# Loading each piece of expert weights in two partition halves, each behind a wait on TensorE's progress

## What is computed

```python
def _attn_ref(r, k, v, w, u):          # (4, 8, 768, 48)
    state = zeros((B, H, D, D))
    for t in range(S):
        cur = einsum('bhd,bhe->bhde', u[None] * kt, vt)
        y[:, :, t] = einsum('bhd,bhde->bhe', rt, state + cur)
        state = w[None, :, :, None] * state + einsum('bhd,bhe->bhde', kt, vt)

def _moe_ref(x, phi, w1, w2):          # x (3072, 384), 8 experts, 4 slots each, F = 1024
    logits = x @ phi
    slot_input = softmax(logits, over tokens).T @ x
    slot_out[e] = relu(slot_input[e] @ w1[e]) @ w2[e]
    return softmax(logits, over slots) @ slot_out

def _moe2_ref(x, w_in, w_out):         # d_ff = 2048
    h = x @ w_in
    return max(0.01 * h, h) @ w_out
```

## Time and profile before

| | us |
|---|---|
| median of 3 runs | 419.22 |
| the runs | 416.3 to 419.42 |
| the profiled execution | 414.55 |
| its span, from the first to the last instruction | 412.8 |
| mean granted clock of TensorE, share of full speed | 0.962 |

### The profile page before, as it was taken

The page is one execution under the profiler, slowest core; times in us unless marked ns, Lnnn a source line. Parts: engine busy times, 40 slices in busy tenths (PEclk is TensorE's granted clock), DMA queues, the critical chain, the costliest instruction groups (busy, mean ns, idle before and its releaser), DMA issues.

```text
span 412.8 us, 11083 instructions
## 1 busy us (share of the span) xinstructions
PE 393.9 (95%) x4307; PEld 358.3 (87%) x4307; DVE 252.5 (61%) x435; ACT 230.3 (56%) x601; POOL 58.2 (14%) x73
## 2 busy tenths in 40 slices
PE   8799998989996899989999999999999999999996
PEld 8788998989995344359999999999999999999995
DVE  7987985579863520177856555555555565555553
ACT  5556554256653224767865565565565555655652
POOL 5445453335530100000000000000000000000000
PEclk9789997599999799989999999999999999999999
DMA  7989998689987998900001010010010010100101
GB/s 170 266 247 300 271 272 237 172 244 274 254 302 276 389 402 325 417 32 2 0 2 57 2 57 1 2 57 2 0 58 0 3 54 1 59 0 2 57 2 57
DMA packets 16253, 54.95 MB, mean 133 GB/s; under 512 B 2640, under 2 KB 6224, under 8 KB 15184
## 3 DMA queue, kind: packets, MB, share of 16 engines
q1 hardware_dynamic: 16064, 54.27, 40.6%
q10 hardware_dynamic: 144, 0.05, 0.0%
HBM read 49.60 MB, written 4.72 MB: 132 GB/s over the span
## 4 chain that ended last, share of the span: by engine, by line
PE 91%; issue 3%; DVE 2%; ACT 1%; DMA 1%; SPq 0%; POOL 0%; ACTq 0%; POOLq 0%
PE ps L1009 17%; PE ps L1014 17%; PE ps L1010 16%; PE ps L776 6%; PE ps L987 5%; PE ps L819 5%; PE ps L813 4%; PE ps L797 3%; PE ps L946 3%; PE ps L786 3%; PE ps L927 3%; PE ps L843 2%; PE ps L833 2%; PE ps L890 2%; DMA rk<-rk_t 1%
## 5 line engine op out<-in xcount | busy, mean ns | idle before, releaser
L1009 PE MATMUL ps<-w_hi,g_hi 128*128 128x384 f32 x384 | 131.8, 343 | 0.7 <-ACT g_hi L750 0.7
L1010 PE MATMUL ps<-w_lo,g_hi 128*128 128x384 f32 x384 | 130.0, 339 | 0.0
L603 DVE SCALAR_TENSOR_TENSOR g_full<-h_full 128x384 f32<-128x384 f32 x128 | 71.5, 558 | 89.4 <-ACT h_full L741 89.2
L750 ACT ACTIVATE g_hi<-g_full 128x384 fp32r<-128x384 f32 x128 | 67.3, 526 | 74.4 <-DVE g_full L603 74.0
L1014 PE MATMUL ps<-w_hi,g_lo 128*128 128x384 f32 x384 | 89.2, 341 | 0.0
L1009 PEld LDWEIGHTS ps<-w_hi,g_hi 128*128 128x128 f32 x384 | 72.2, 188 | 1.7 <-ACT g_hi L750 1.0
L1010 PEld LDWEIGHTS ps<-w_lo,g_hi 128*128 128x128 f32 x384 | 72.4, 189 | 0.5 <-issue 0.5
L592 DVE TENSOR_TENSOR g_lo<-g_full,g_hi 128x384 fp32r<-128x384 f32 x128 | 70.5, 551 | 0.1
L741 ACT ACTIVATE h_full<-ps 128x384 f32<-128x384 f32 x128 | 62.4, 487 | 14.4 <-PE ps L987 4.0
L1014 PEld LDWEIGHTS ps<-w_hi,g_lo 128*128 128x128 f32 x384 | 69.6, 189 | 0.0
L661 ACT ACTIVATE bonus_v<-nat,bonus 128x48 f32<-128x48 f32 x192 | 46.0, 322 | 0.8
(11 more groups left out here) (120 smaller groups left out, 354.2 us busy)
## 6 DMA issues: line engine op xcount, KB each, us to landing
w_units<-early_pieces SPq DMA_DIRECT2D x24, 512.0 KB, 6.5
rk<-rk_t SPq DMA_DIRECT2D x48, 192.0 KB, 3.9
nat<-rkv SPq DMA_DIRECT2D x20, 384.0 KB, 5.6
m_unit<-late_units SPq DMA_DIRECT2D x3, 1536.0 KB, 7.1
x_unit<-late_units SPq DMA_DIRECT2D x3, 1536.0 KB, 9.8
out<-y_out SPq DMA_DIRECT2D x7, 576.0 KB, 3.0
w_units<-late_units SPq DMA_DIRECT2D x2, 1536.0 KB, 8.5
m_unit<-w_in SPq DMA_DIRECT2D x4, 768.0 KB, 10.8
```

The lines of the kernel that those rows point to most:

```text
L603: dve.scalar_tensor_tensor(out=g_full[:, f % 2], in0=h_full[:, f % 2], scalar=0.01, in1=h_full[:, f % 2], op0=ALU.mult, op1=ALU.max).then_ ...
L750: act.activation(g_hi[:, f % 4], g_full[:, f % 2], ACT.Copy).then_inc(g_hi_done, 1)
L1009: pe.matmul(bank, g_hi[:, f % 4, bass.ts(s, P)], w_hi[:, f], start=(f == 0), stop=False)
L1010: pe.matmul(bank, g_hi[:, f % 4, bass.ts(s, P)], w_lo[:, f], start=False, stop=False)
```

## The change

A piece is no longer loaded by one DMA on 128 partitions but by two, for partitions 0 to 63 and for 64 to 127, of 256 KB each. In iteration i SP waits ahead of the first half until PE has finished the scores of step i-3, and ahead of the second until it has finished the bonus sums of step i-3. The four pieces after the loop are issued as eight halves without waits. The count for which the first expert waits is doubled, and nothing else changes.

```diff
-            def load_piece(n):
-                sp.dma_start(pieces[:, bass.ts(n, PIECE)], early_pieces[n]).then_inc(early_loaded, 16)
+            def load_piece(n, half):
+                rows = slice(HALF * half, HALF * half + HALF)
+                sp.dma_start(pieces[rows, bass.ts(n, PIECE)], early_pieces[n, rows]).then_inc(early_loaded, 16)
...
                 if i >= RK_BUFS:
-                    load_piece(i - RK_BUFS)
+                    sp.wait_ge(scores_ready, i - 2)
+                    load_piece(i - RK_BUFS, 0)
+                    sp.wait_ge(bonus_ready, i - 2)
+                    load_piece(i - RK_BUFS, 1)
             for n in range(STEPS + 1 - RK_BUFS, 3 * EARLY):
-                load_piece(n)
+                load_piece(n, 0)
+                load_piece(n, 1)
...
-                        pe.wait_ge(early_loaded, 16 * 3 * EARLY)
+                        pe.wait_ge(early_loaded, 16 * 6 * EARLY)
```

## The result

The changed kernel takes 439.0 us (median of 4 runs, 434.51 to 441.92) where the kernel before takes 418.13 (4 runs, 416.3 to 419.42): a ratio of 1.0467, 95% interval 1.0358 to 1.0575. By the medians that is 20.9 us more. Measured again later beside other kernels it was 435.46 (6 runs) to 418.53 (11 runs), a ratio of 1.0428 (1.0329 to 1.0527). The profiled execution of the changed kernel took 441.92 us and is the longest of its runs, the one of before took 414.55, so the two traces are 27.4 us apart and not 20.9.

A forecast was written before the change was run, and what follows sets the result against it. PE bound the kernel, with DMA transfers nearly as limiting in the recurrence. 24 us of extra transfers less 17.0 idle and 0.7 slack left 6.3 us, on the runs' median 419.22 rounded down to 425 us; range 414 to 436.

The forecast's parts named there:

- Extra issues and waits: On SP in the recurrence: 24 more DMA issues, 10.3 us under 57.8 us of waits, and two new waits; cost nothing.
- Price of a half: Each piece loaded as two 64-partition halves takes 1.0 us more DMA time, 24 us for all 24 pieces.
- Slack of rk: In the recurrence rk has 7.1 us slack; transfers 7.8 us late by 64 us stretch it by 1 to 2 us.
- What hides it: From 20 to 160 us, 17.0 us of idle DMA time absorb part of 24 us extra, leaving 7.0 us late.
- w_in: Last quarter of w_in, read at L967, has 0.7 us slack; of transfers 7.0 us late, 6.3 us reach PE.
- Hidden: Rival: the halves' extra DMA time is wholly hidden; 419 us, chance 0.28.
- The late instruction load: Rival: PE's 1.55 us stall at 64.21 us and the clock fall behind it vanish, worth 7.9 us; 411 us, chance 0.12.
- Low clock: Rival: PE's waits for rk in the recurrence bring two more clock falls, 12.8 us on top; 438 us, chance 0.10.

The follow-up runs named there:

- the waits alone: Kernel before with both new waits ahead of each piece, still one whole load: 422.47 us to 420.76, ratio 1.0125; measured again 421.62 to 419.2.
- loads alone: A kernel with all computation left out, timing loads in several partition and column forms: eight whole pieces 12.5 us, in partition halves 20.2.
- every other piece: Changed kernel with only every other piece in halves, the other 12 whole behind the first wait: 434.08 us to 418.53 before, ratio 1.0472.
- rk in one load: rk loaded by one DMA on 128 padded partitions instead of two of 48: kernel before 421.28 us (ratio 1.0028), changed kernel 435.7 us (1.0494).

## Why the prediction was right and wrong

*Forecast.* The direction was right; 425 us, or 6.3 us over before, was less than a third of the 20.9 measured, and the range ended at 436 (439.0 measured, 435.46 the second time).

*Extra issues and waits.* Right within what can be told. SP still waits at L275 for 36.6 us, and the waits alone moved the medians by about 2 us, which isn't told from nothing.

*Price of a half.* Right: 1.0 us for a piece was taken, 0.96 is measured with loads alone. In the recurrence itself the window 44 to 64 fell from 281 to 212 GB/s, 4.66 to 6.18 us for 1.31 MB, though the kernel was at other steps then. The estimate from the figure of the Trainium skill ("SBUF — State Buffer", section "Door 1: The DMA port swizzle", about 218 GB/s for 64 partitions) was 1.06, and the loads alone agree with it within a tenth (0.96).

*Slack of rk.* Wrong as a path. VectorE was to wait at its scaling from about 64 us, because the transfers would be 7.8 us late there. It waited once, for 0.4 us, in the first 20 us and not there. The landings of rk grew from a median of 3.9 to 5.5 us, by far less than the slack of 7.1.

*What hides it.* The step that failed: "Together 17.0 us" of idle DMA time set against 24 us of extra transfers. It counts only data whose reader comes late. The instruction blocks of PE run over the same engines, and a block that is late stalls PE at once, however much idle DMA time comes later. With half of the extra time (every other piece), which this step hides entirely, the loss was still about 16 us, 9 of them at a like clock. In the two traces the unexplained stalls of PE grew from 3.5 to 13.6 us. On top of them the changed kernel ran at a lower clock, about 6 us, which the forecast's sum put at nothing.

*w_in.* The wait came, the way to it was another: L972 waited for w_in by 2.3 us in the list of waits, where 6.3 less the recurrence's part had been put there. It was to come from transfers that are 7.0 us late. But the loads of w_in wait for PE's own products, and PE reached the first expert 23.4 us late, so they were issued 23.4 us later than before (179.4 us after 156.0). What was left is that the longest of them landed after 15.6 instead of 12.8 us.

*Rivals.* Hidden: refuted as a whole. The late instruction load: the place was seen and the sign was wrong. I asked only whether one of them could vanish, and wrote myself that longer transfers make it later; that sentence was the mechanism of the loss and deserved a price. The Trainium skill's "Runtime: NRT & Kernel Launch", section "Instruction fetch mechanics", calls these fetches mostly hidden. At 31 ns a matmul and beside loads they are not: up to 3.35 us at a block. Low clock: its 438 us is close to the 439.0 measured, and that is luck. It was to follow from waits for rk, of which there were none, and to cost 12.8 us; by the estimate above the clock is about 6 us.

Open: why a block takes 8.7 us beside a full queue when its own packet lasts 1.3 us; whether the blocks ride on one engine that could be spared; why rk in one load gives nothing back; why the changed kernel runs at a lower clock. No version here beats the kernel before.

## What to carry to other kernels

Loads that stayed on one side of partition 64 took 1.5 to 1.8 times as long as the same bytes in loads that span both sides (22.6 us to 14.7 and to 12.5); to split a load, split its columns, or don't split it. Where PE runs through unrolled code of small matmuls beside heavy loads, look for stalls that end shortly behind a packet of the instruction queue: the DMA engines' spare time is then no allowance, since instructions need it at once. An idle share that is summed over a whole stage says nothing for a reader that needs its data within a few microseconds. And before a loss is put down to one cause, compare runs at the same granted clock.

## What the runs showed of the hardware that I had not expected

- A block of 256 PE instructions came every 3.9 us when there were no loads (12.5 blocks in 49.3 us, PE's own pace), every 6.2 us beside whole pieces and every 8.7 beside partition halves.
- Sixteen loads of 64 partitions took 14.7 us as partitions 32 to 95 and 22.6 us as partitions 0 to 63.
- The granted clock was 0.50 to 0.52 from 20 to 44 us in eight of the thirteen profiled executions, 0.72 in one and 0.86 to 1.00 in four, with PE busy for 23 to 24 of the 24 us in the low ones.
- A matmul of 2 columns into one half of the output partitions came every 107 ns, and one of 48 columns every 62 ns, or every 31 ns when the two halves of the output took turns, all at a granted clock of 1.00.
